# Attention and two gated products on one core: heads in pairs with seven tiles of 128 query rows, and a softmax pipeline in half-unit steps

## What is computed

```python
scores = cap * tanh((q @ k.T) / sqrt(64) / cap)
attn = softmax(scores)                    # 4 x 12 heads, 448 x 448
x = (attn @ v) -> [1792, 768]             # heads side by side
x = (sigmoid(x @ w_gate) * (x @ w_val)) @ w_out       # 768 -> 1536 -> 768
h = x @ w_in                                          # 768 -> 2048
y = (h * cos(h)) @ w_out2                             # 2048 -> 768
```

## Time and profile before

| | us |
|---|---|
| median of three runs | 1310.38 (1307.38 to 1311.06) |
| profiled execution | 1308.7 |
| its span, first to last instruction | 1306.9 |
| TensorE busy | 1266.8 |
| VectorE busy | 716.9 |
| ScalarE busy | 569.1 |
| GpSimd busy | 400.4 |

### The profile page before, as it was taken

One profiled execution on the slowest core, in us unless ns is written; L12 is line 12 of the kernel. 1 busy time (PEld: TensorE's weight loads), 2 busy tenths in 40 slices (PEclk: granted clock), 3 DMA queues, 4 the chain that ended last, 5 costly groups with the idle time before them and its releaser, 6 DMA issues.

```text
span 1306.9 us, 17361 instructions
## 1 busy us (share of the span) xinstructions
PE 1266.8 (97%) x6468; PEld 1138.3 (87%) x6468; DVE 716.9 (55%) x1249; ACT 569.1 (44%) x1085; POOL 400.4 (31%) x394
## 2 busy tenths in 40 slices
PE   7899998999899999999999999999999999999999
PEld 5557997889888999999999999999999999999998
DVE  6993438868887312786676511487667621113620
ACT  5881135545654212665665311566565411103610
POOL 4526887758976001340042000341022100000000
PEclk8999999999999999999999999999999999999999
DMA  3327896658865567654675366754685456666673
GB/s 96 82 80 262 326 326 239 204 193 303 321 245 222 199 217 246 201 166 166 231 253 194 132 224 227 239 176 147 218 283 179 151 196 217 217 218 217 228 243 127
DMA packets 115812, 274.84 MB, mean 210 GB/s; under 512 B 32784, under 2 KB 35856, under 8 KB 115728
## 3 DMA queue, kind: packets, MB, share of 16 engines
q1 hardware_dynamic: 112128, 268.22, 59.6%
q10 hardware_dynamic: 3600, 5.51, 1.1%
HBM read 214.70 MB, written 58.98 MB: 209 GB/s over the span
## 4 chain that ended last, share of the span: by engine, by line
PE 84%; DVE 9%; ACT 4%; issue 2%; DMA 0%; POOL 0%; POOLq 0%; ACTq 0%
PE acc L421 23%; PE acc L422 23%; PE acc L423 23%; PE t_ps L360 5%; DVE prob L714 3%; PE s_ps L351 3%; PE s_ps L352 3%; PE acc L369 2%; PE acc L370 2%; ACT prob L554 2%; PE acc L383 1%; DVE tmp_b L810 1%; DVE rowmax L702 1%; DVE tmp_b L807 1%; DVE h_lo L819 1%
## 5 line engine op out<-in xcount | busy, mean ns | idle before, releaser
L421 PE MATMUL acc<-h_hi,w_hi 128*128 128x448 f32 x672 | 256.9, 382 | 0.0
L422 PE MATMUL acc<-h_lo,w_hi 128*128 128x448 f32 x672 | 246.8, 367 | 0.0
L423 PE MATMUL acc<-h_hi,w_lo 128*128 128x448 f32 x672 | 246.6, 367 | 0.0
L421 PE MATMUL acc<-x_hi,w_hi 128*128 128x448 f32 x576 | 210.7, 366 | 0.0
L422 PE MATMUL acc<-x_lo,w_hi 128*128 128x448 f32 x576 | 210.4, 365 | 0.0
L423 PE MATMUL acc<-x_hi,w_lo 128*128 128x448 f32 x576 | 210.4, 365 | 0.0
L785 DVE TENSOR_TENSOR tmp_b<-acc,tmp_a 128x448 f32<-128x448 f32 x48 | 30.0, 624 | 229.8 <-PE acc L423 229.6
L554 ACT ACTIVATE prob<-prob,shift,cap_abs 112x448 f32<-112x448 f32 x192 | 144.1, 752 | 5.1 <-DVE shift L704 4.5
L421 PE MATMUL acc<-z_hi,w_hi 128*128 128x448 f32 x384 | 140.3, 365 | 1.0 <-DVE z_lo L797 1.0
L423 PE MATMUL acc<-z_hi,w_lo 128*128 128x448 f32 x384 | 140.2, 365 | 0.0
L422 PE MATMUL acc<-z_lo,w_hi 128*128 128x448 f32 x384 | 140.2, 365 | 0.0
(11 more groups left out here) (77 smaller groups left out, 2018.3 us busy)
## 6 DMA issues: line engine op xcount, KB each, us to landing
w_hi<-w_pair SPq DMA_DIRECT2D x156, 384.0 KB, 3.0
w_lo<-w_pair SPq DMA_DIRECT2D x156, 384.0 KB, 3.8
qk_raw<-qk SPq DMA_DIRECT2D x48, 448.0 KB, 4.9
w_raw<-w SPq DMA_DIRECT2D x52, 384.0 KB, 4.7
w_pair<-w_hi SPq DMA_DIRECT2D x52, 384.0 KB, 2.3
w_pair<-w_lo SPq DMA_DIRECT2D x52, 384.0 KB, 3.3
w_hi<-w_pair SPq DMA_DIRECT2D x36, 512.0 KB, 3.3
w_lo<-w_pair SPq DMA_DIRECT2D x36, 512.0 KB, 4.5
```

Of the source, the lines that this page charges most:

```text
L421: e.matmul(out[:, 0:S], w_hi[p][:, wb, :], a_hi[:, kb, :], start=first, stop=False)
L422: e.matmul(out[:, 0:S], w_hi[p][:, wb, :], a_lo[:, kb, :], start=False, stop=False)
L423: return e.matmul(out[:, 0:S], w_lo[p][:, wb, :], a_hi[:, kb, :], start=False, stop=last)
```

## The change

The kernel is rewritten around pairs of heads. What it does:

- Two heads side by side have 896 query rows, seven tiles of 128; tile 3 holds the last 64 rows of the first head and the first 64 of the second. q_hl has 64 zero columns between the heads, and the straddling tile is computed by four matmuls, two with each head's k, that add up in one bank.
- The seven tiles make four groups, (0, 1), (2, 3), (4, 5), (6). A step of the pipeline is one group, and lies beside one half-unit of the second or fourth product. Scores run AHEAD = 4 groups before the group's own step. The first four groups of a batch lie beside the last two units of the first product.
- Keys lie in chunks of 128, 128, 128 and 64. In the last one, v's 64 rows are stored twice (the host repeats them), the high part of the probabilities goes to partitions 0 to 63 of pt_hi and the low part to 64 to 127: one matmul does both. VectorE's low part is two instructions for a tile.
- In the heads alone, tiles 1 and 5 of seven are copied by ScalarE and the other five by VectorE; keys stay in four chunks of 112. The first product's first units are issued between the last steps.
- w_raw has one buffer for each half instead of two, and SyncE's order is by halves: load a half, store the half before. GpSimd waits for each half alone.
- v is loaded and split in chunks of 128; prob is one buffer of seven tiles, q_hl one for both heads, scratch buffers are shared. The additions of credits to semaphores at the start are gone.
- ScalarE and VectorE take a unit's result out of PSUM at the start of the next unit, ahead of its heads' parts.

The core of the diff:

```diff
-QT = 112
+TILES = 7
+GROUPS = ((0, 1), (2, 3), (4, 5), (6,))
+NG = len(GROUPS)
+GAP = P - S % P
+CH = 3
+BY_SCALAR = (1, 5)
+AHEAD = NG
...
-    w_raw = [[sb(f"w_raw{p}{h}", [P, HALF_MAX, P]) for h in range(2)] for p in range(2)]
+    w_raw = [sb(f"w_raw{h}", [P, HALF_MAX, P]) for h in range(2)]
...
+    prob = sb("prob", [P, TILES, S])
+    pt_hi = sb("pt_hi", [P, CH + 1, 2 * S], F32R)
+    pt_lo = sb("pt_lo", [P, CH, 2 * S], F32R)
...
+            def load_raw(stage, j, h):
+                u, w = unit_no(stage, j), {1: w1, 2: w2, 3: w3, 4: w4}[stage]
+                if u > 0:
+                    e.wait_ge(s_wsplit, 2 * (u - 1) + h + 1)
+                e.dma_start(w_raw[h][:, 0:BLK[stage], :], w[j, h, :, :, :]).then_inc(s_wld[h], 16)
...
+                            if b == 0:
+                                if unit_no(stage, j) > 0:
+                                    load_raw(stage, j, h)
+                                if before:
+                                    keep(*before)
+                                before = (stage, j, h)
...
+            def scores(g, to):
...
+                    if t == CH:
+                        for d in range(2):
+                            q = q_hl[:, q_at(t) + d * GAP:q_at(t) + d * GAP + P]
+                            e.matmul(out, q, k_hh[d][:, :], start=(d == 0), stop=False)
+                            m = e.matmul(out, q, k_ll[d][:, :], start=False, stop=(d == 1))
...
+            def transposes(g):
+                for x in tiles_of(g):
+                    bank_is_free(x)
+                    e.wait_ge(s_norm, x + 1)
+                    for c in range(CH):
+                        e.transpose(t_ps[x % 2][:, bass.ts(c, P)], prob[:, x % TILES, bass.ts(c, P)], ident[:, :])
+                    m = e.transpose(t_ps[x % 2][0:D, bass.ts(CH, P)], prob[:, x % TILES, CH * P:S], ident[:, :])
+                    m.then_inc(s_tr, 1)
...
+            def times_v(b, i, d):
...
+                for c in range(CH + 1):
+                    vv = v_hl[d][:, c, :, :].rearrange("p a d -> p (a d)")
+                    m = e.matmul(o_ps[d][:, 0:S], vv, pt_hi[:, c, d * S:(d + 1) * S], start=(c == 0), stop=(c == CH))
+                    if c < CH:
+                        e.matmul(o_ps[d][:, 0:S], vv, pt_lo[:, c, d * S:(d + 1) * S], start=False, stop=False)
...
+            def attend(b, n, blocks):           # TensorE
+                i, r = divmod(n, NG)
+                if n + AHEAD < STEPS:
+                    g = group_of(b, n + AHEAD)
+                    e.wait_ge(s_tanh, g)
+                    scores(g, s_ps)
+                blocks(0)
+                if 0 <= n + 1 < STEPS:
+                    transposes(group_of(b, n + 1))
+                blocks(1)
+                if i >= 0 and r in (1, 3):
+                    times_v(b, i, r // 2)
+                blocks(2)
...
+            for m in range(2, STEPS + 1):
+                alone(m)
+            gate_or_value(0, 0, 0, (0, 1, 2))
+            alone(STEPS + 1)
+            gate_or_value(0, 0, 0, (3, 4))
+            alone(STEPS + 2)
+            gate_or_value(0, 0, 1, (0, 1, 2, 3, 4))
+            alone(STEPS + 3)
+            gate_or_value(0, 1, 0, (0, 1, 2, 3, 4))
...
+            def attend(b, n):                   # ScalarE
+                if n > 0:
+                    if n + AHEAD - 1 < STEPS:
+                        exp(group_of(b, n + AHEAD - 1))
...
+                if n + AHEAD < STEPS:
+                    tanh(group_of(b, n + AHEAD))
...
+                if 0 <= n + 1 < STEPS:
+                    pt_high(group_of(b, n + 1))
...
+            def attend(b, n):                   # VectorE
+                if n + AHEAD < STEPS:
+                    row_max(group_of(b, n + AHEAD))
+                if 0 <= n + 1 < STEPS:
+                    pt_low(group_of(b, n + 1))
...
+                if i >= 0 and r in (0, 2) and n != 2 * U2:
+                    output(pair_of(b, i), r // 2)
...
+                if n > 0:
+                    if n + AHEAD - 1 < STEPS:
+                        normalise(group_of(b, n + AHEAD - 1))
...
+            def alone(m):                       # VectorE
+                if m < STEPS:
+                    row_max(m)
+                if 0 <= m - 3 < STEPS:
+                    pt_copies(m - 3)
+                if 0 <= m - 1 < STEPS:
+                    normalise(m - 1)
```

1165 lines of the change are left out of this document (597 added, 568 removed).

## The result

The changed kernel takes 1344.94 us (median of 4 runs, 1343.40 to 1351.59) against 1309.16 for the kernel before on the same chip: a ratio of 1.028, 95% interval 1.024 to 1.032. The prediction said 1272, range 1255 to 1297, and was wrong in its sign.

What follows compares the result with a forecast made beforehand. TensorE's own work was taken to bound batches 1 to 3, VectorE the heads alone, with 28.3 us of excess in batch 0. 1306.9 - 12.8 - 5.5 - 18.3 = 1270.3 us of span, plus 1.8: 1272 us, range 1255 to 1297.

Steps and rivals of the forecast that it cites:

- Heads alone: Stretch before the first product: 3 us less VectorE work, 4 us from draining, 1.5 us startup cost; net gain 5.5 us.
- VectorE is dense: Heads alone: VectorE's work of 16.3 us for two heads, six times from 9.5 us on, gives 107.
- the drain: End of heads alone: 45 first-product matmuls (9.1 us) put between the last softmax steps; 4 us gained.
- The startup bubble: Start of heads alone: second group of rows needs the second head's split, ended at 11.3 us; 1.5 us lost.
- Weights: Batch 0: store, load and split of a half take 7.9 us against 7.29, with 8.1 of lead; 2 us lost.
- Rival (b): Batch 0's first and third products: single raw buffer decides if a lone load lands in 7 us; 1322 us, chance 0.06.
- Batch 0's excess: Batch 0's 28.3 us over 306.7: waits for normalised rows and tanh go, 10 us stay; gain 18.3 us.
- what is late next is VectorE's mere throughput: Batch 0's second product: VectorE needs 24.4 us a pair against TensorE's 23.7; 4 us of the excess left there.
- TensorE's work beside the products: Every pair of heads: fewer matmuls save 0.41 us, transposes 0.30; 0.71 x 18 pairs = 12.8 us gained.
- near 302 with TensorE never idle: Sign of a right forecast: batches 1 and 2 near 302 us or below for 306.7, TensorE never idle.
- 2 at the boundaries of products: Batch 0: 2 us of the excess left where z_low of the last unit stands behind an output on VectorE.
- rival (c): All three batches with heads: an engine handover waits every half-unit, 0.5 us in 72 steps; 1308 us, chance 0.06.

Runs made afterwards that it cites:

- the run with all gains but the late scores: Changed kernel with P times V late, one more ScalarE copy, two raw buffers, earlier q and k splits, scores of steps 1 and 13 not moved: 1316.12 us, ratio 1.006.
- the last one: Same gaining edits on the changed kernel, plus ScalarE's tanh ahead of exponentials and group 2's exponentials in step -2 at the second product: 1310.70 us, ratio 1.002.

## Why the prediction was wrong, point by point

**Heads alone, -5.5 predicted.** The failed step is "VectorE is dense" carried over to the new order. The sum of VectorE's work was good (85.36 us busy; 87.47 before), and the drain did take the work that was meant for it. But the sum holds only while VectorE is fed, and I had not asked where the fp32 products with V stand in TensorE's queue. In place of the term: +13.5 us counting the moved matmuls, by the fastest profile; 1.3% of the whole, some 15 to 18 us (1344.94 to 1329.57 by the medians, 1.0283 to 1.0149 by the ratios), comes back by their order and a copy. With these, the first product matmul is at 99.5 us, and "before 105" holds there and in six of the seven later runs with both edits. The term for the copies is small in the runs too, and they can't tell it from nothing. The startup bubble was there and larger than the 1.5 us: the first two row maxima start at 11.3 and 14.7 us (9.5 and 11.2 before), so the second is 3.5 us later.

**Weights, 2 us predicted, bounds 0 and 15.** The chain was right (7.9 us, of 7.9), the lead was not, in three ways. First, by my own numbers ten units of 0.6 us and two splits of q and k of 3.6 are 13.2 us, which 8.1 us of lead do not cover; I wrote "close" and took 2. In the runs these splits lengthen the chain's turns. Second, the single buffer allows no split ahead of its load, so the lead is never built up again once it is used, and the third product, for which the sum has no term at all, pays like the first. On the kernel before, with this edit alone, the first three products lose 8.8, 4.4 and 7.5 us, 19 in the whole (16 to 22 by the ratio's interval), beyond my upper bound. Third, in the changed kernel the lead isn't there to begin with: 1.8 us at unit 2. Two buffers take 14.6 us off batch 0 there, and 0.5% off the whole. Rival (b), "the single raw buffer decides", came true in part by another road: I tied it to a landing of over 6.4 us, but the loads landed in 4.1 (the page's median), and the buffer cost all this nevertheless.

**Batch 0's excess, -18.3 predicted.** The mechanism was right: TensorE's waits for low parts and tanh inside batch 0's last three products went from 15.3 us to 1.7. The step "what is late next is VectorE's mere throughput" failed: VectorE is busy for 69.99 of 80.0 us in the second product, and what is late is GpSimd's split of q and k, 13.9 us in three waits. In this part of the sum I had written of these splits only that their loads are spread. The second to fourth products take 236.6 us in the changed kernel for 239.9 before, 233.0 with two raw buffers, and 230.5 with the splits half a unit earlier besides, since the wait that goes comes back in part as one for tanh. They take 229.0 us in the run with all gains but the late scores and 226.9 in the last one, so 11 to 13 of the 18 us could be had.

**TensorE's work beside the products, 4.3 us less a batch (0.71 x 6 pairs).** 30 matmuls of 448 columns a pair instead of 32 came as said. The transposes were mis-sized:

```profile
694.24 0.49 PE L373 MATMUL t_ps<-ident,prob 128*128 128x128 f32 x3
...
695.02 0.45 PE L411 MATMUL acc<-h_hi,w_hi 128*128 128x448 f32 x1
```

Eight of 128 columns take 695.02 - 694.24 = 0.78 us where eight of 112 took 0.70: 0.098 and 0.088 us each, a ratio of 1.11 for one of 1.14 in columns. They are paid nearly by column, the bound I had set at 0.41 us a pair, and nothing was won on them. The Trainium skill (TensorE: Matmul & The Clock Gate, section Part 4: PE-mode transpose) gives about 275 ns for one, in the context of one kernel, and a fixed latency as most of it. The record lasts that long here too (mean 273 ns in batch 1), but queued ones start 0.098 us apart, and it is the pitch that a sum must use.

**Batches 1 and 2, "near 302 with TensorE never idle".** They take 313.1 and 315.0. For batch 1 against 306.6: twelve matmuls less, -2.4; waits of 3.7 us for tanh and 1.5 for normalised rows, +5.2; the low clock after them, +1.2 at the second product; and the matmuls of the third product start 0.2067 us apart for 0.2026, +1.2. That is 5.2 of the 6.5 seen; the other 1.3 us I can't place. The failed step is "2 at the boundaries of products", sized for batch 0 alone and by z_low; the same boundary stands in every batch with heads, and its price is a wait for tanh, or for normalised rows when ScalarE's or TensorE's order is turned. The edits on these orders alone did not shorten it, so what exactly makes the boundary late is not shown by a run. It is a relative of rival (c), but tanh is waited for at four places and not in 72 steps; in the steady state the handover has its slack, until VectorE's order is turned.

**Sum.** I took the gains from the waits that were removed, each by itself, and gave all that might be late next to one engine. The range held none of the places where the time went, because its ends were built from the sizes of the terms I had, and not from terms I lacked.

## What to carry to other kernels

For each queue write down what stands directly in front of the instruction that feeds the loop which sets the pace, and how long it takes; a block of 2.7 us there cost 1.1% of the whole, more than all the work that was saved. A buffer taken away is priced at pace, chain against consumption, over every unit and with all that the same engine does in between, and a lead counts only if something builds it up again. Where hand-made exceptions for the first steps of a stage are replaced by one uniform rule, price the boundary once for each stage and batch, and move one instruction at a time: turning one engine's order in all steps cost 80 us where a wait in one step was meant.

## What the runs showed that was not expected

Two multiplications on VectorE that take 0.82 us at 585.44 us take 2.48 and 2.50 when they meet GpSimd's subtraction of k and q, not only that of weights:

```profile
579.84 2.48 DVE L753 TENSOR_SCALAR prob<-prob,recip 128x448 f32<-128x448 f32 x2
585.44 0.82 DVE L753 TENSOR_SCALAR prob<-prob,recip 128x448 f32<-128x448 f32 x2
...
603.87 2.50 DVE L753 TENSOR_SCALAR prob<-prob,recip 128x448 f32<-128x448 f32 x2
```

```profile
579.67 1.14 POOL L268 TENSOR_TENSOR k_ll<-qk_raw,k_hh 128x448 fp32r<-128x448 f32 x1
580.89 1.18 POOL L268 TENSOR_TENSOR q_hl<-qk_raw,q_hl 64x448 fp32r<-64x448 f32 x1
```

The first pair ends at 582.32 us, just behind GpSimd's second subtraction (582.07). The Trainium skill's lock between the two engines (SBUF — State Buffer, section Who interferes with whom), cited in the prediction for the weights, agrees with this for the smaller work too. VectorE had the time to spare here: TensorE waits for nothing between 568.4 and 699.4 us.

The pitch of product matmuls in the third product of batches 1 and 2 of the changed kernel was 0.2067 us instead of 0.2026, and it fell back about the next wait of TensorE. No run was made for its cause, and it stays open. So does what the last version still lacks in batch 1 against the kernel before, 312.2 us for 306.6, with 5.5 us of waits of TensorE for normalised rows and tanh: 1.1 at the end of the first product, 3.3 at the start of the second and 1.2 at that of the fourth.
